# Low parts of attention's inputs and of the first layer's weights made on GpSimd, and g held in its PSUM bank

## What is computed

```python
def sm_attn(qq, kk, vv):
    s = scale * np.matmul(qq, kk.transpose(0, 1, 3, 2))
    s = s - np.max(s, axis=-1, keepdims=True)
    a = np.exp(s)
    a = a / (np.sum(a, axis=-1, keepdims=True) + 1e-09)
    return np.matmul(a, vv)
p_packed = sm_attn(p, k, v)              # 8 batches, 8 heads, 32 packed rows
x = sm_attn(q, p_packed, p_packed)       # 576 rows of 64, as 4608 tokens x 512
h = x @ w_in                             # 512 -> 2048
g = np.maximum(h, 0.0) + alpha * np.minimum(h, 0.0)
y = g @ w_out                            # 2048 -> 512
gate = y @ w_gate                        # 512 -> 1536
out = (gate / (1 + np.exp(-gate)) * (y @ w_val)) @ w_down
```

## Time and profile before

| | us |
|---|---|
| median of 3 runs | 1597.93 (1597.17 to 1599.99) |
| profiled execution | 1597.42 |
| its span, first to last instruction | 1595.2 |
| busy TensorE, VectorE, ScalarE, GpSimd | 1562.7, 1148.5, 728.5, 76.3 |

### The profile page before, as it was taken

How to read it: one execution, slowest core, us unless ns; L and a number is a source line. 1 busy time by engine, 2 the same in 40 slices (tenths; PEclk the granted TensorE clock), 3 DMA queues, 4 the chain that set the end, 5 groups by cost and what they waited for, 6 DMA issues and landing times.

```text
span 1595.2 us, 24866 instructions
## 1 busy us (share of the span) xinstructions
PE 1562.7 (98%) x9330; PEld 1436.2 (90%) x9330; DVE 1148.5 (72%) x2010; ACT 728.5 (46%) x1475; POOL 76.3 (5%) x123
## 2 busy tenths in 40 slices
PE   8999999999999999999999999999999999999999
PEld 5899988989999999999988888888888889999998
DVE  5777679868698687987865577556765685667666
ACT  4565568555685656745532144223412252233223
POOL 0000000100001000014300000000000000000000
PEclk9999999999999999999999999999999999999999
DMA  7343225523345233338665665766667667877856
GB/s 269 111 126 115 79 73 161 166 87 120 115 123 178 65 131 121 98 147 293 213 219 192 238 212 178 245 235 217 192 213 237 215 200 248 300 271 238 290 203 218
DMA packets 132502, 293.15 MB, mean 184 GB/s; under 512 B 13456, under 2 KB 41120, under 8 KB 132384
## 3 DMA queue, kind: packets, MB, share of 16 engines
q1 hardware_dynamic: 120544, 249.08, 49.0%
q0 software_dynamic: 11840, 42.48, 7.0%
HBM read 239.61 MB, written 51.90 MB: 183 GB/s over the span
## 4 chain that ended last, share of the span: by engine, by line
PE 80%; DVE 13%; ACT 3%; issue 2%; DMA 1%; ACTq 0%; DVEq 0%
PE acc L986 9%; PE side L778 9%; PE side L779 9%; PE side L780 9%; PE h L778 8%; PE h L780 8%; PE h L779 8%; PE acc L990 5%; PE acc L778 5%; PE acc L780 4%; PE acc L779 4%; DVE piece L1441 3%; DVE mixed L1441 2%; DVE floats L1633 2%; DVE g L1441 1%
## 5 line engine op out<-in xcount | busy, mean ns | idle before, releaser
L986 PE MATMUL acc<-g,w 128*128 128x288 f32 x1792 | 272.4, 294 | 0.0
L986 PEld LDWEIGHTS acc<-g,w 128*128 128x128 f32 x1792 | 249.0, 188 | 0.0
L1119 ACT ACTIVATE g<-floats 128x288 fp32r<-128x288 f32 x256 | 113.8, 444 | 223.3 <-DVE floats L1633 152.5
L1441 DVE TENSOR_TENSOR g<-floats,g 128x288 fp32r<-128x288 f32 x256 | 115.2, 450 | 68.0 <-ACT g L1119 66.5
L1323 ACT ACTIVATE rows_b<-side 128x512 f32<-128x512 f32 (+1 forms) x60 | 33.4, 557 | 285.6 <-PE side L780 285.6
L1441 DVE TENSOR_TENSOR piece<-floats,piece 128x512 fp32r<-128x512 f32 (+3 forms) x217 | 143.5, 682 | 25.2 <-ACT piece L1119 22.5
L778 PE MATMUL h<-attn,mixed 128*128 128x288 f32 x512 | 157.8, 308 | 3.5 <-DVE floats L1633 2.1
L1633 DVE SCALAR_TENSOR_TENSOR floats<-floats,h 128x288 f32<-128x288 f32 x256 | 130.4, 509 | 39.9 <-ACT floats L1276 38.3
L990 PE MATMUL acc<-g,w 128*128 128x288 f32 x896 | 156.2, 296 | 0.2 <-DVE g L1441 0.2
L780 PE MATMUL h<-attn,mixed 128*128 128x288 f32 x512 | 151.3, 295 | 0.0
L779 PE MATMUL h<-attn,mixed 128*128 128x288 f32 x512 | 151.2, 295 | 0.0
(11 more groups left out here) (284 smaller groups left out, 3810.5 us busy)
## 6 DMA issues: line engine op xcount, KB each, us to landing
ring<-w_scratch SPq DMA_DIRECT2D x90, 512.0 KB, 4.4
wring<-d_scratch SPq DMA_DIRECT2D x168, 256.0 KB, 2.9
ring_c<-w_scratch SPq DMA_DIRECT2D x60, 512.0 KB, 4.1
w_scratch<-piece POOLq DMA_DIRECT2D x36, 512.0 KB, 4.0
floats<-w_in SPq DMA_DIRECT2D x64, 256.0 KB, 3.2
ring_b<-w_scratch SPq DMA_DIRECT2D x30, 512.0 KB, 4.8
d_scratch<-piece POOLq DMA_DIRECT2D x42, 256.0 KB, 3.8
ring<-d_scratch SPq DMA_DIRECT2D x42, 256.0 KB, 3.0
```

The lines of the kernel that those rows point to most:

```text
L986: pe.matmul(acc[:, m, 0:CH], w2[:, j, x, m * P:(m + 1) * P], g[:, s % 2, 0, :], start=False, stop=False)
L1119: return nc.scalar.activation(dst, src, ACT.Copy, **kw)
L1441: return nc.vector.tensor_tensor(dst, x, high.bitcast(F32), ALU.subtract)
```

## The change

The low parts of pieces of k, v, q, w (w_in) and o (w_out) are made by GpSimd (`input_low`), in the order of `PLAN`, each counted in a new semaphore `input_split`. VectorE keeps the low parts of the second layer's weights (`weight_low`). `low_of(p)` says which semaphore and value stand for a piece; loads, TensorE and stores wait on it. relu(-h) goes to an SBUF tile `minus`; VectorE writes gF back into the bank `hb`, and both `g_hi` and `g_lo` read it there, so h(s+2) waits for `g_split` instead of `gF_done`.

```diff
@@ -285,6 +285,9 @@
 
 PIECES = [e[1] for e in PLAN if e[0] == "split"]
 PIECE_NO = {p: n for n, p in enumerate(PIECES)}
+
+BY_POOL = [p for p in PIECES if p[0] in "kvqwo"]
+BY_DVE = [p for p in PIECES if p[0] in "gs"]
 RAWS = [p for p in PIECES if p[0] != "s"]
 RAW_NO = {p: n for n, p in enumerate(RAWS)}
 AHEAD = RAW_NO["g", EARLY_KEEPS - 1, 0]
@@ -376,7 +379,7 @@
         packT = packT_[:, :].rearrange("p (x h i n) -> p x h i n", x=2, h=2, i=2)
         both = both_[:, :].rearrange("p (x h i n) -> p x h i n", x=2, h=2, i=2)
 
-        gF = f(2304, 576).rearrange("p (s n) -> p s n", s=2)
+        minus = f(2304, 576).rearrange("p (s n) -> p s n", s=2)
         ystage = f(2880, 1152).rearrange("p (m n) -> p m n", m=KD)
         nmax1, sum1, rec1, eps1 = f(4032, 2), f(4034, 2), f(4036, 2), f(4038, 2)
         max2, sum2, rec2 = f(4040, 18), f(4058, 18), f(4076, 18)
...
@@ -561,6 +565,10 @@
             return (f(4224, 1024) if j < EARLY_KEEPS else late_sums[:, :])
 
 
+        def low_of(p):
+
+            return (input_split, BY_POOL.index(p) + 1) if p in BY_POOL else (piece_split, BY_DVE.index(p) + 1)
+
         def unsplit(p):
 
             return weight_sums(p[1])[:, 512 * p[2]:512 * p[2] + 512] if p[0] == "s" else raw(p)
@@ -586,7 +594,7 @@
 
             def load(p):
                 if RAW_NO[p] >= RING:
-                    once.wait_ge(piece_split, PIECE_NO[RAWS[RAW_NO[p] - RING]] + 1)
+                    once.wait_ge(*low_of(RAWS[RAW_NO[p] - RING]))
                 dst = raw(p)
                 if p[0] == "k":
                     src = kT[p[1], p[2], :, :]
...
@@ -733,6 +741,15 @@
         @block.gpsimd
         def _(pool):
             once = Once(pool)
+            def input_low(p):
+                k, c = piece_rows(p), piece_columns(p)
+                once.wait_ge(input_split, BY_POOL.index(p))
+                once.wait_ge(both0_zeroed, 1)
+                once.wait_ge(packF_zeroed, before(("split", p), "clear") + 1)
+                once.wait_ge(piece_high, PIECE_NO[p] + 1)
+                nc.gpsimd.tensor_tensor(piece(p)[k, 1, c], unsplit(p)[k, c], piece(p)[k, 0, c].bitcast(F32), ALU.subtract
+                                        ).then_inc(input_split, 1)
+
             pool.dma_start(alphas, alpha).then_inc(alpha_landed, 16)
             nc.gpsimd.memset(ident, 0.0).then_inc(ident_zeroed, 1)
             once.wait_ge(ident_zeroed, 1)
@@ -743,15 +760,18 @@
             once.wait_ge(t1_done, 2)
             nc.gpsimd.memset(f(4224, 512), 0.0).then_inc(both0_zeroed, 1)
             for e in PLAN:
-                if e[0] == "clear":
+                if e[0] == "split" and e[1] in BY_POOL:
+                    input_low(e[1])
+                elif e[0] == "clear":
                     if e[1] == 1:
                         once.wait_ge(pT_done, 2)
                     else:
                         once.wait_ge(packT_done, e[1] - 1)
+                    once.wait_ge(input_split, sum(p in BY_POOL for p in PIECES[:before(e, "split")]))
                     nc.gpsimd.memset(f(7104, 512), 0.0).then_inc(packF_zeroed, 1)
                 elif e[0] == "keep":
                     p = pieces_of(e)[0]
-                    once.wait_ge(piece_split, PIECE_NO[p] + 1)
+                    once.wait_ge(*low_of(p))
                     if e[1] >= NT2:
                         for s in range(1 if e[2] == 0 else 2):
                             pool.dma_start(dS[e[1] - NT2, e[2], s], piece(p)[:, :, 256 * s:256 * s + 256].bitcast(F32)
@@ -958,7 +978,7 @@
                     once.wait_ge(attn_split, 2 * b + c + 1)
                 if c == 0 and j % 4 == 0:
                     once.wait_ge(mix_split, mixed_by(b, j // 4))
-                once.wait_ge(gF_done, s - 1)
+                once.wait_ge(g_split, s - 1)
                 for half in range(2):
                     mm = product(hb[s % 2][:, 0:CH], hl(lambda x: mixed[:, b % 2, x, half, j * P:(j + 1) * P]),
                                  hl(lambda x: attn[:, x, half, c * CH:(c + 1) * CH]), half == 0, half == 1)
...
@@ -1272,13 +1292,14 @@
 
             def neg(s):
                 once.wait_ge(h_done, s + 1)
-                once.wait_ge(g_split, s - 1)
-                nc.scalar.activation(gF[:, s % 2, :], hb[s % 2][:, 0:CH], ACT.Relu, scale=-1.0).then_inc(neg_done, 1)
+                once.wait_ge(gF_done, s - 1)
+                nc.scalar.activation(minus[:, s % 2, :], hb[s % 2][:, 0:CH], ACT.Relu, scale=-1.0
+                                     ).then_inc(neg_done, 1)
 
             def g_hi(s):
                 once.wait_ge(gF_done, s + 1)
                 once.wait_ge(y_done, s - 1)
-                copy(g[:, s % 2, 0, :], gF[:, s % 2, :]).then_inc(g_high, 1)
+                copy(g[:, s % 2, 0, :], hb[s % 2][:, 0:CH]).then_inc(g_high, 1)
 
             def y_copy(c):
                 once.wait_ge(y_stored, 16 * c)
...
@@ -1440,11 +1461,10 @@
             def subtract(dst, x, high):
                 return nc.vector.tensor_tensor(dst, x, high.bitcast(F32), ALU.subtract)
 
-            def split(p):
-                n = PIECE_NO[p]
-                k, c = piece_rows(p), piece_columns(p)
-                once.wait_ge(piece_high, n + 1)
-                subtract(piece(p)[k, 1, c], unsplit(p)[k, c], piece(p)[k, 0, c]).then_inc(piece_split, 1)
+            def weight_low(p):
+                c = piece_columns(p)
+                once.wait_ge(piece_high, PIECE_NO[p] + 1)
+                subtract(piece(p)[:, 1, c], unsplit(p)[:, c], piece(p)[:, 0, c]).then_inc(piece_split, 1)
 
             def sums(e):
 
...
@@ -1630,13 +1650,14 @@
                 once.wait_ge(neg_done, s + 1)
                 once.wait_ge(nalpha_ready, 1)
                 j = s % NT1
-                nc.vector.scalar_tensor_tensor(out=gF[:, s % 2, :], in0=gF[:, s % 2, :], scalar=alphas[:, j:j + 1],
-                                               in1=hb[s % 2][:, 0:CH], op0=ALU.mult, op1=ALU.add
+                nc.vector.scalar_tensor_tensor(out=hb[s % 2][:, 0:CH], in0=minus[:, s % 2, :],
+                                               scalar=alphas[:, j:j + 1], in1=hb[s % 2][:, 0:CH],
+                                               op0=ALU.mult, op1=ALU.add
                                                ).then_inc(gF_done, 1)
 
             def g_lo(s):
                 once.wait_ge(g_high, s + 1)
-                subtract(g[:, s % 2, 1, :], gF[:, s % 2, :], g[:, s % 2, 0, :]).then_inc(g_split, 1)
+                subtract(g[:, s % 2, 1, :], hb[s % 2][:, 0:CH], g[:, s % 2, 0, :]).then_inc(g_split, 1)
 
             def y_copy(c):
                 once.wait_ge(y_stored, 16 * c)
@@ -1785,8 +1806,8 @@
                     attn_0(e[1])
                 elif e[0] == "alpha":
                     alpha_1()
-                elif e[0] == "split":
-                    split(e[1])
+                elif e[0] == "split" and e[1] in BY_DVE:
+                    weight_low(e[1])
                 elif e[0] == "split_p":
                     split_p(e[1])
                 elif e[0] == "max1":
...
```

13 lines of the change are left out of this document (7 added, 6 removed).

## The result

The changed kernel takes 1608.8 us (median of 4 runs, 1607.97 to 1609.8), the kernel before 1598.41 us on the same chip (1597.17 to 1599.99). The ratio is 1.0065, 95% interval 1.0047 to 1.0082: the change makes the kernel slower, by some 10 us. The forecast of 1601 us was too low, and so, by 0.8 us, was the upper end of its range, 1608. The profiled execution took 1609.8 us, of which the span is 1608.0.

The account below looks back on a forecast made before the run. TensorE was taken to bound the kernel, with VectorE setting the pace for about a seventh of the time. The sum was 1597.4 - 6.5 + 3.4 + 6.5 = 1600.8, stated as 1601 us, range 1591 to 1608 us.

Parts of the forecast that it names:

- What bounds the kernel: Whole span: TensorE busy 98%; the change can win only within TensorE's 21 idle us before 720 us.
- Relief, -6.5 us: TensorE's waits for VectorE before 720 us: moving 171 low parts off VectorE shortens them by 6.5 us.
- late k pieces, +3.4: Near 326, 570 and 579 us: GpSimd's low parts reach TensorE late, 3 x 1.1 + 0.1 = 3.4 us.
- the first rival: Before 820 us: relief reaches further, two thirds of 18.8 us go and half of g_lo's lateness; 1591 us, chance 0.25.
- The bank, +6.5 us: First layer: h(s+2) waits for g_lo(s) instead of gF(s), about 0.9 us later; costs 6.5 us.
- My list of pairs of h(s+2) and g_lo(s): All 254 pairs compared; in 44, g_lo(s) ended only after h(s+2) had started; charges sum to 6.5 us.
- the other late ones vanish: Late g_lo not charged have a moved piece in the run ahead of them, so their lateness goes; no cost.
- A low part on GpSimd at 1.15 us: GpSimd's subtraction of 512 columns: 1.15 us assumed, between 0.54 and 1.63; 1.2 us for 576 columns.
- Nothing for contention: The sum to 1601 us charged nothing for GpSimd and VectorE holding each other up when both read SBUF.
- my second rival: K pieces and softmax: low part 1.6 us or more, or GpSimd and VectorE contend over SBUF; 1606 us, chance 0.20.
- Signs in the profile: Profile after: VectorE busy 115 to 125 us less, h waits for g_lo 6 us, waits naming GpSimd 5 to 6.
- the three things that I had named as showing me wrong: No h wait for g_lo from 690 to 820 us, low part above 1.5 us, or longer two-input VectorE instructions.

Follow-up runs that it names:

- Fills of nearly that length: Changed kernel with each GpSimd low part replaced by two zero fills and g kept in SBUF, h waiting for gF alone: 1591.16 us, ratio 0.9957.
- two fills: Changed kernel, g still in its bank, with each GpSimd low part replaced by two fills with zeros: 1598.17 us, ratio 1.0005.
- three fills: Changed kernel with each GpSimd low part replaced by three fills with zeros: 1608.62 us, ratio 1.0067.
- fills as long: Changed kernel with each GpSimd low part replaced by two zero fills and a short third, as long as the subtraction: 1602.0 us, ratio 1.0026.
- the bank alone: Kernel before with g held in its PSUM bank and h waiting for g_lo, all low parts on VectorE: 1609.56 us, ratio 1.0077.

## Why the prediction was wrong

*What bounds the kernel.* Right. All that the change did happened before 820 us, and VectorE's waits were what it moved. The second layer kept its length (791 us from the start of h(255) in both).

*Relief, -6.5 us, and late k pieces, +3.4.* Together I had -3.1 us for pieces of 1.15 to 1.2 us. Fills of nearly that length gave -6.9, 4 us more, and the trace of that kernel shows it in both terms. It is 5.2 us ahead at slot 58, where my list of waits had about 2 us by then: the relief reached further than the runs of VectorE that I went through, as the first rival said, though not by the 6 us that it named for the pieces, let alone with g_lo in time. And at the three places of k pieces (h(88), h(168) and h(171)) it loses 0.44, 0.44 and 0.39 us, where I had 1.1 each.

*The bank, +6.5 us.* Right in kind and nearly in size: +7.7 beside the relief, uncertain by 2.7. My list of pairs of h(s+2) and g_lo(s) is what carried it. It named the stretches as well (slots 118, 214 and 252 each jumped by about 1.0 to 1.6 us). With every piece left on VectorE the bank costs 12 us, as more pairs are late then. But "the other late ones vanish" was wrong: of the 44 late pairs 30 are still late with every moved piece off VectorE, among them g_lo of slots 73, 84 and 85 by 1.0 to 1.5 us, none of which is in my list of charges. And single places were too low: I gave 1.1 us to four of them together, at 301 and three others, and the wait at 300.44 shown above is 1.43 us alone.

*A low part on GpSimd at 1.15 us.* This step failed first. I took two fills and a little from a bracket of 0.54 to 1.63 us; the subtraction took 1.30 and 1.47. The Trainium skill (GPSIMD Engine Reference, section 3.1) gives 4497 ns for 2048 elements; the estimate of 1.12 us for 512, a quarter of it, was too low here as well. The step from 1.1 to 1.3 us cost 3.4 us. I had written that 1.63 us would give about 6 us in place of 3.4 in all; three fills of 1.7 us showed 9.9 us more than two fills, of which the clock may have a part. The latency of a k piece is not the only thing that grows: between slots 56 and 72, where w pieces are made in pairs for a mixing of weights, three fills lost 2.9 us against two (shifts -4.0 and -3.8 at slot 56, -1.9 and -4.6 at slot 72); a stretch of 3.4 us at half the clock, from 258.7 us, falls in there too. They lost another 3 between slots 160 and 176, with no such stretch.

*Nothing for contention.* This is the larger miss, 6.2 us. It was my second rival, with a chance of 0.20, and its mechanism was right: VectorE's instructions with two SBUF inputs grew longer and those with a PSUM operand didn't. I priced it as 24 us of VectorE's time of which TensorE feels 3. It was less of VectorE's time: its busy time is 1060.4 us in the change and 1047.7 with fills as long, 12.7 less, of which 11 are the 44 pieces by 97 ns and 15 softmax steps each by 219 and 240 ns. But TensorE felt 6 of the 12.7, one half, where I had an eighth. Steps like these stand in the bursts in which TensorE waits for VectorE, which would explain it; how much of each is on the path was not measured. The 6.2 us also hold what GpSimd's own 11 held subtractions cost, 3.8 us of its time in all. And I counted them against the busy time rather than against the runs ahead of each wait, which I had done for the relief.

With 3.4 raised to 6 and 3 added, this rival came to 1606 us, the nearest of the forecasts.

*The range.* The length, the contention and the bank were off by 3.4, 6.2 and 1.2 us to the slower side, the relief and late k pieces by 4 to the faster; that the miss is 8 us and not some 11 is luck. The bounds of the low part were added as 3 us, but they should have been joined with the contention, since both grow with the time that GpSimd spends on a piece.

*Signs in the profile.* VectorE's busy time fell by 88 us, not by 115 to 125. Only 13 of the missing us are longer instructions; with fills as long, which hold up nothing, it fell by 101, because neighbours overlap: my own 0.60 us for each of 171 pieces gives 103. VectorE's two-input instructions grew, one of the three things that I had named as showing me wrong; the low part's 1.47 us for 576 columns came close to a second, 1.5. The waits for g_lo did appear, 14 to 15 us of them; some were waits for something else before. Waits naming GpSimd are only 2.9 us, since a late piece mostly shows as a wait for what comes after it (`mixed`, 2.5 us in two waits).

**Still open.** How the 6.2 us of the reads divide among pieces of g and s, softmax steps and sums was not tried. Nor was a real subtraction with g in SBUF and GpSimd's reads timed to miss g_lo. Why the clock falls in some executions and not in others was not tried, and so not whether it belongs to the cost of the change. TensorE's busy time is 5 us longer in the changed kernel than before. The two stretches at half the clock can make up to 3.4 of them; the bank alone has 1566.1 without any such stretch, and the first matmul after a wait has the longer record (0.37 us at 300.44, against 0.29), so part of it may be the waiting, but nothing measured that by itself.

## What to carry to other kernels

Before elementwise work goes to GpSimd, list VectorE's instructions with two SBUF inputs that run beside it: each can be held until GpSimd's instruction ends, and keeping one operand in PSUM frees it (0.447 us against 1.175 for g_lo). Freeing a buffer later is cheap only where the later event is early; compare the two events pair by pair, and switch the scheme on only for the stretch where it wins. An average (busy time freed) says little: 121 us moved gave 7 us even with fills that hold up nothing, and 59 of the 171 pieces, moved in the stretch where the bank could be held for nothing, gave 5.

## What the runs showed of the hardware

- A GpSimd subtraction of two SBUF inputs takes 1.30 us for 512 columns, 1.29 with 64 partitions, and 1.43 for 576 (1.47 on average, with those that are held up); VectorE takes 0.69 and 0.75. A fill on GpSimd takes 0.53 us (512), 0.58 (576), 0.21 (128) and 0.15 (64).
- A VectorE instruction with two SBUF inputs that begins while GpSimd subtracts is over a fixed time after that subtraction ends: 0.31 to 0.33 us for 288 columns (58 g_lo), 0.61 or 0.62 for 576 (13 softmax steps). The other way round, all 11 subtractions of over 1.45 us, up to 1.92, began while such an instruction ran.
- Beside GpSimd's subtractions g_lo (288 columns, both inputs in SBUF) took 652 ns on average over the kernel and 710 in the early part; with one input in PSUM 450, and beside fills, which read nothing, 451 with both in SBUF:

```profile
L1464 DVE TENSOR_TENSOR g<-floats,g 128x288 fp32r<-128x288 f32 x256 | 115.3, 451 | 81.5 <-ACT g L1142 80.0
```

- VectorE's write of 288 columns into PSUM costs 9 ns more than into SBUF (518 and 509), and its read from PSUM nothing; ScalarE copies 33 ns faster from PSUM (411 and 444).
